# A fused attention and two MLPs in one kernel: the end of the attention, the first chunk of the first MLP, and the order inside an attention slot

## What is computed

```python
# q, k, v: (4, 8, 576, 64), s: (4, 8, 576)
scores = q @ k.T / sqrt(64)
cum    = cumsum(max(s, 0))
scores = where(causal, -1e9, scores + min(-(cum_i - cum_j), 0))
attn   = exp(scores - max) / (sum + 1e-9) @ v         # (4, 8, 576, 64)
x = attn as (2304, 512)
h = x @ w_in;  g = h - tanh(h);  x = g @ w_out         # w_in 512x2048, w_out 2048x512
h = x @ w2_in; solu = h * softmax(h)                   # w2_in 512x1024
out = layernorm(solu) * g_ln @ w2_out                  # w2_out 1024x512
```

## Time and profile before

| | us |
|---|---|
| median of 3 runs (lowest, highest) | 890.28 (888.71, 890.87) |
| the profiled execution | 890.16 |
| its span in the profile | 888.3 |
| PE busy | 851.2 (96%) |
| DVE busy | 445.8 (50%) |
| ACT busy | 381.2 (43%) |
| POOL busy | 104.1 (12%) |

### The profile page before, as it was taken

The page is one execution under the profiler, slowest core; times in us unless marked ns, Lnnn a source line. Parts: engine busy times, 40 slices in busy tenths (PEclk is TensorE's granted clock), DMA queues, the critical chain, the costliest instruction groups (busy, mean ns, idle before and its releaser), DMA issues.

```text
span 888.3 us, 14439 instructions
## 1 busy us (share of the span) xinstructions
PE 851.2 (96%) x4800; PEld 738.0 (83%) x4800; DVE 445.8 (50%) x1047; ACT 381.2 (43%) x856; POOL 104.1 (12%) x134
## 2 busy tenths in 40 slices
PE   4899999999979899999999999999999999999998
PEld 3788888888878678888888888899998888888886
DVE  4677877877743435222422322242565655544553
ACT  3777777777633334222322322232542433333332
POOL 2222222222100000000000000000003222112210
PEclk9899999999999999999999999999999999999999
DMA  6444444454303222000000000000210000000000
GB/s 153 120 123 122 121 128 128 118 141 112 117 31 95 71 95 95 1 1 1 0 0 0 0 0 0 0 0 1 60 36 0 25 24 24 12 24 24 24 24 35
DMA packets 77713, 46.28 MB, mean 52 GB/s; under 512 B 59824, under 2 KB 68144, under 8 KB 77680
## 3 DMA queue, kind: packets, MB, share of 16 engines
q1 hardware_dynamic: 77680, 45.86, 18.3%
HBM read 40.97 MB, written 4.87 MB: 52 GB/s over the span
## 4 chain that ended last, share of the span: by engine, by line
PE 78%; DVE 6%; DMA 4%; ACT 4%; issue 4%; SPq 1%; DVEq 0%; ACTq 0%
PE psum L1024 19%; PE psum L1011 19%; PE psum L1190 11%; PE psum L1218 11%; PE psum L1091 5%; PE psum L1051 4%; DMA stage<-in_moe_w_out 4%; PE psum L1119 4%; PE psum L1204 2%; PE psum L1055 1%; DVE probs L813 1%; ACT pT_hi L582 1%; DVE w1i L772 1%; DVE pT_lo L796 1%; ACT w1i L559 1%
## 5 line engine op out<-in xcount | busy, mean ns | idle before, releaser
L1011 PE MATMUL psum<-x_hi,w1i 128*128 128x464 f32 (+1 forms) x640 | 186.7, 373 | 4.8 <-DVE w1i L772 4.8
L1011 PEld LDWEIGHTS psum<-x_hi,w1i 128*128 128x128 f32 x640 | 120.8, 189 | 19.4 <-issue 3.5
L1011 PE MATMUL psum<-x_lo,w1i 128*128 128x464 f32 (+1 forms) x320 | 119.5, 373 | 0.0
L902 DVE TENSOR_TENSOR gate_lo<-gate,gate_hi 128x464 fp32r<-128x464 f32 (+1 forms) x80 | 51.1, 638 | 104.2 <-ACT gate_hi L667 103.4
L893 DVE TENSOR_TENSOR gate<-psum,gate 128x464 f32<-128x464 f32 (+1 forms) x80 | 51.0, 637 | 99.4 <-ACT gate L657 99.2
L667 ACT ACTIVATE gate_hi<-gate 128x464 fp32r<-128x464 f32 (+1 forms) x80 | 47.1, 588 | 113.0 <-PE psum L1024 102.3
L591 ACT ACTIVATE probs<-probs,neg_max 128x128 f32<-128x128 f32 (+2 forms) x144 | 83.8, 582 | 22.1 <-DVE neg_max L813 21.9
L1218 PE MATMUL psum<-w2o,lnT_hi 128*128 128x512 f32 x288 | 92.2, 401 | 0.5 <-DVE lnT_lo L971 0.5
L657 ACT ACTIVATE gate<-psum 128x464 f32<-128x464 f32 (+1 forms) x80 | 44.2, 553 | 109.4 <-PE psum L1011 107.3
L1024 PE MATMUL psum<-gate_hi,w1o_hi 128*128 128x464 f32 (+1 forms) x320 | 80.6, 373 | 8.1 <-DVE gate_lo L902 8.1
L582 ACT ACTIVATE pT_hi<-psum 128x512 fp32r<-128x512 f32 (+3 forms) x160 | 64.9, 438 | 42.9 <-PE psum L1119 42.9
(11 more groups left out here) (111 smaller groups left out, 1346.1 us busy)
## 6 DMA issues: line engine op xcount, KB each, us to landing
cum_bc<-cum_dram SPq DMA_DIRECT2D x16, 576.0 KB, 4.3
rden_T<-rden_dram SPq DMA_DIRECT2D x32, 144.0 KB, 2.9
out_x<-out_sb SPq DMA_DIRECT2D x18, 256.0 KB, 2.0
stage<-in_q SPq DMA_DIRECT2D x32, 128.0 KB, 2.3
stage<-in_k SPq DMA_DIRECT2D x32, 128.0 KB, 2.4
v_raw<-in_v SPq DMA_DIRECT2D x32, 128.0 KB, 3.6
stage<-in_moe_w_in SPq DMA_DIRECT2D x16, 256.0 KB, 2.7
stage<-in_moe_w_out SPq DMA_DIRECT2D x16, 256.0 KB, 3.0
```

Source lines behind the costliest of these rows:

```text
L902: dve.tensor_tensor(gate_lo[j % 2][:, 0:n], gate[j % 2][:, 0:n], gate_hi[j % 2][:, 0:n].bitcast(F32), ALU.subtract).then_inc(gate_lo_done, 1)
L1011: mm = pe.matmul(h_ps[j % 4][:, 0:wide(c)], wp[j][:, kt, :], xp[:, kt, 0:wide(c)], start=(n == 0), stop=(n == 3 * KT - 1))
```

## The change

The order and place of work change; what is computed does not.

- **Beginning.** k of pair 0 is issued from ACT's queue; SP issues s, q0, then cum's store, q1, the wait, cum_bc of pair 0, k1. DVE clears only the parts of `stage` ahead of the cumulative sums, the rest behind them. PE waits for four increments of dve_const. In slot -1 the three parts of q and k turn in three banks.
- **Slot order.** PE: `score(2)` ahead of `turn_rden`, `turn_qk(0)`. ACT: `exp(1, 0)`, `exp(1, 1)` ahead of `rden_rows_copy`, `qk_copy(0)`. DVE: `qk_rest(0)` behind `bias(0, 2)`, `bias(1, 2)`; `bias(None, FULL)` ahead of `qk_rest(2)`.
- **X_CUT** from 256 to 128.
- **Chunk 0.** `AHEAD = 4`. x of chunk 0 is split in halves at the ends of slots 14 and 15 (`first_x`); the four w_in tiles inside slot 16 (`first_w1i`); up(0, 0..3) inside and behind slot 16 (`first_up`). PE then runs down(j-4), up(j). step(0, 0) does not wait for the last x_mult. Steps 0 to 3 split two w_out tiles each, later ones tile j+4, and w_in tile j+3 behind gate_hi and gate_lo. The two halves of `stage` have a semaphore each; SP reloads each half by itself.
- Memory is laid out anew: `probs`, `qkT_hi`, `qkT_lo` and `cum_bc` come first, and the gates and the first w_out tiles lie on them.

```diff
-        AHEAD = 3
+        AHEAD = 4
-        HALF, X_CUT = S // 2, 2 * P
+        HALF, X_CUT = S // 2, P
+        def w1o_at(j):
+            return range(2 * j, 2 * j + 2) if j < AHEAD else range(j + AHEAD, min(j + AHEAD + 1, FT))
+        def qk_bank(sl, n):
+            return bank((5, 4, 3)[n]) if sl.fixed and sl.s < 0 else qk_ps
...
 # SP
-            for n in range(2):
-                load_qk(n, n)
+            load_tokens(sp, q_raw[0], q_pairs, 0, qk_in[0], diagonal=True)
             sp.wait_ge(cum_step, 3)
             sp.dma_start(cum_dram, cum8).then_inc(cum_out, 16)
+            load_tokens(sp, q_raw[1], q_pairs, 1, qk_in[1], diagonal=True)
             sp.wait_ge(cum_out, 16)
...
+                if sl.fixed and sl.s == -1:
+                    load_tokens(sp, k_raw[1], k_pairs, 1, qk_in[1])
                 if sl.fixed and sl.s == PAIRS - 1:
                     sp.wait_ge(turned_qk, 3 * PAIRS)
-                    for j in range(4):
-                        load_w1(j)
+                    for j in range(2):
+                        load_w1i(j)
...                                       # rden_T of this slot
+                if sl.fixed and sl.s == PAIRS - 1:
+                    for j in range(2, 4):
+                        load_w1i(j)
+                    for j in range(4):
+                        load_w1o(j)
...
             for j in range(4, FT):
+                sp.wait_ge(w1i_lo_done, j - 3)
+                load_w1i(j)
                 sp.wait_ge(w1o_lo_done, j - 3)
-                load_w1(j)
+                load_w1o(j)
...
 # ACT (DVE in the same places, with the lo parts)
+            load_tokens(act, k_raw[0], k_pairs, 0, qk_in[0])
+            def first_x(sl):
+                if sl.fixed and sl.s in (PAIRS - 2, PAIRS - 1):
+                    act.wait_ge(x_done, HALVES)
+                    split_x(0, (0, 1) if sl.s == PAIRS - 2 else (2, 3))
...
-            act.wait_ge(attended, 2 * PAIRS)
-            act.wait_ge(x_done, PAIRS)
+            act.wait_ge(turned_p, UNITS * PAIRS)
+            act.wait_ge(v_split, 2 * PAIRS)
             for j in range(FT):
+                if j == 1:
+                    act.wait_ge(x_done, PAIRS)
                 step(0, j)
...
 # DVE, end of a slot
                 p_lo("B2")
+                bias(None, FULL)
                 qk_rest(2)
-                bias(None, FULL)
+                first_w1i(sl, 3)
                 p_lo("B3")
-                ahead(sl)
+                first_x(sl)
+                if sl.fixed and sl.s == LAST:
+                    step(0, 0)
+                    x_mult()
...
 # PE
-            pe.wait_ge(dve_const, 2)
+            pe.wait_ge(dve_const, 4)
...
+                if weights:
+                    for j in range(AHEAD, FT):
+                        down(c, j - AHEAD, weights)
+                        up(c, j, weights)
+                    for j in range(FT - AHEAD, FT):
+                        down(c, j, weights)
...
                 turn_p("A2")
+                score(2)
                 turn_rden()
                 turn_qk(0)
-                score(2)
...
                 turn_qk(1)
+                if sl.fixed and sl.s == PAIRS:
+                    first_up(0)
...
                 attend(-1, 0, 1)
+                if sl.fixed and sl.s == PAIRS:
+                    first_up(1)
                 turn_p("B3")
                 attend(-1, 0, 2, 3, 4)
                 if sl.fixed and sl.s == PAIRS:
-                    pe.wait_ge(biased, TILES * PAIRS)
-                    up(0, 0, True)
+                    first_up(2)
             attention(pe, slot)
-            for j in range(1, AHEAD):
-                up(0, j, True)
+            first_up(3)
```

More of the change, by code:

```diff
@@ L165, in build_transformer @@
             gate_lo = [sb(f"gate_lo{n}", [P, CH], F32R) for n in range(2)]
+            w1o = sb("w1o", [P, FT, 2, DM], F32R)
+            w1o_hi, w1o_lo = ([w1o[:, j, part, :] for j in range(FT)] for part in range(2))
             sb("pad1", [P, pad])
@@ L191, in build_transformer @@
             w2o = sb("w2o", [P, FT2, 2, DM], F32R)
[L192 removed]
+            w2o_hi, w2o_lo = ([w2o[:, (f - AHEAD) % FT2, part, :] for f in range(FT2)] for part in range(2))
             y_hi = [sb(f"y_hi{n}", [P, KT, P], F32R) for n in range(2)]
@@ L225, in build_transformer @@
         stage_in = [sem(f"stage_in{n}") for n in range(4)]
+        w1o_in = [sem(f"w1o_in{n}") for n in range(4)]
         g_in = sem("g_in")
@@ new lines, in w2o_lo_part, with step @@
+            def w2o_lo_part(n):
+                for f in (2 * n, 2 * n + 1):
+                    dve.wait_ge(w2o_hi_done, f + 1)
+                    dve.scalar_tensor_tensor(out=w2o_lo[f][:, :], in0=stage[n][:, (f % 2) * DM:(f % 2 + 1) * DM],
+                                             scalar=g_col[:, f:f + 1], in1=w2o_hi[f][:, :].bitcast(F32),
+                                             op0=ALU.mult, op1=ALU.subtract).then_inc(w2o_lo_done, 1)
+            def step(c, j):
+                u = FT * c + j
+                dve.wait_ge(tanh_done, u + 1)
+                n = wide(c)
+                dve.tensor_tensor(gate[j % 2][:, 0:n], h_ps[j % 4][:, 0:n], gate[j % 2][:, 0:n],
+                                  ALU.subtract).then_inc(gate_done, 1)
+                if isinstance(c, int) and c == 0:
+                    for m in w1o_at(j):
+                        w1o_lo_part(m)
+                if isinstance(c, int) and c == NCH - 1 and FT2 <= j < FT2 + KT:
+                    w2i_lo_part(j - FT2)
+                if isinstance(c, int) and c == NCH - 1 and j >= FT2 + KT:
+                    w2o_lo_part(j - FT2 - KT)
+                dve.wait_ge(gate_hi_done, u + 1)
+                dve.tensor_tensor(gate_lo[j % 2][:, 0:n], gate[j % 2][:, 0:n], gate_hi[j % 2][:, 0:n].bitcast(F32),
+                                  ALU.subtract).then_inc(gate_lo_done, 1)
+                if isinstance(c, int) and c == 0 and 0 < j <= FT - AHEAD:
+                    w1i_lo_part(j + AHEAD - 1)
@@ L789, in slot, with first_x, first_w1i @@
+            def first_x(sl):
+                if sl.fixed and sl.s in (PAIRS - 2, PAIRS - 1):
+                    split_x(0, (0, 1) if sl.s == PAIRS - 2 else (2, 3))
+            def first_w1i(sl, j):
+                if sl.fixed and sl.s == PAIRS:
+                    w1i_lo_part(j)
             def slot(sl):
@@ L856, in slot @@
                 p_lo("A2")
-                qk_rest(0)
                 bias(0, 2)
                 bias(1, 2)
+                qk_rest(0)
+                first_w1i(sl, 0)
                 p_lo("A3")
-                x_mult()
+                if not (sl.fixed and sl.s == LAST):
+                    x_mult()
                 p_lo("T")
+                first_w1i(sl, 1)
                 qk_rest(1)
@@ L908, in copy_y @@
                     dve.tensor_copy(xT[:, m, tokens(c)], y_ps[m][:, 0:wide(c)]).then_inc(y_dve, 1)
-            for j in range(FT):
+            for j in range(1, FT):
                 step(0, j)
```

187 lines of the change are left out of this document (85 added, 102 removed).

## The result

| us | before | after |
|---|---|---|
| median (lowest, highest) | 889.77 (888.71, 890.87), 4 runs | 860.58 (860.31, 860.85), 4 runs |
| the profiled execution | 890.16 | 860.57 |
| its span | 888.3 | 858.7 |
| PE busy | 851.2 (96%) | 839.3 (98%) |

The ratio is 0.967, with a 95% interval of 0.966 to 0.969: 29.2 us less, where 22.6 were forecast. In what follows the spans of the two profiled executions are compared, 29.6 us apart.

What follows compares the result with a forecast made beforehand. PE, busy 96% of the span, was taken as the bound, with waits for gate_lo (8.1 us) and neg_max (7.1) to remove. 890.16 - 17.8 - 4.0 - 1.5 + 0.8 = 867.7 us; range 863.5 to 876.

Steps and rivals of the forecast that it cites:

- End of attention and chunk 0: Slot 16's start to chunk 1's first up: gaps, restart and half clock mostly go, gain 17.8 us, between 15.5 and 19.0.
- the tightest place: up(0, 4) in chunk 0, due at 24.0 with its tile ready at 23.8: 0.2 slack, 0.3 us taken.
- the residue of 1.2: Slot 16 and chunk 0: loss still left after the change, 0.9 us, taken as 1.2 with small latencies.
- Borders: Slot borders: PE's wait of about 0.3 us for neg_max of the tail tile goes, gain 4.0, ends 0 and 4.5.
- The other moves in the slot: Inside the slot: qk_lo(0) about 1.8 us later, rden_rows 1.3 later, both within slack; no gain or cost counted.
- X_CUT: Attends: key tile 1 saves 0.18 us, tile 0 costs 0.14; over 32 heads gain 1.5, ends 0 and 2.5.
- Beginning: Start through slot 0: PE starts about the same, slot 1 near 26.7 instead of 25.89; cost 0.8, ends -0.3 and 2.
- the swap's gain: Slot 0's end: the bias no longer waits behind qk_lo, saving 0.6 us against the new order's cost.
- the cost of the new order: Slot 0: turn_qk(1), at 18.43 before, waits for qk_lo(0) near 20.0 and pushes score(3); 1.4 us in the walk.
- The staging: Rival in chunk 0: SP's in-order queue keeps the 8.1 us of waits for gate_lo, 875.8 us; chance 11%.
- new wait: Rival in the slots: a stall at turn_qk(1) or T, 0.3 us a slot, eats the border gain, 871.7; 13%.
- The beginning did not stay longer at half clock: Rival: a thinner slot 0 moves the half clock past slot 1, +4 us, 871.7 us; chance 4%.

Runs made afterwards that it cites:

- the swap alone: The kernel before with one edit, DVE takes bias(None, FULL) ahead of qk_rest(2): 881.94 us, ratio 0.993.
- the two other traces with before's attention: The kernel before with w_out's parts side by side in memory, 888.73 us; the same with the gates also ahead of w1o, 888.04 us.
- the halves tied: The kernel after, but SP waits for both lo parts of a step before reloading either half of the staging tile: 860.39 us, ratio 0.969.
- the ups behind: The kernel after with up(0,0) to up(0,3) all behind the attention's last matmul, none inside slot 16: 862.24 us, ratio 0.971.
- the run of score(2) alone: The kernel before with score(2) ahead of turn_rden and turn_qk(0), ACT's and DVE's orders moved to match: 885.82 us, ratio 0.998.

## Why the prediction was right and wrong

- **End of attention and chunk 0: -17.8 forecast, -18.6 measured.** The account by waits held, though its parts were not run apart. Slot 16's start to chunk 1's first up is 92.1 (about 93 forecast), no wait for gate_lo or w_in is left, and up(0, 4), called the tightest place, starts at 250.59 with its tile ready near 250.0. Of the residue of 1.2, two waits are seen in slot 16: 0.48 for probs at its start and 0.18 for rden (0.5 and 0.6 forecast). The price of up(0, 4) and the small latencies did not come. One reading was off without harm: the earlier trace rows has ACT and DVE busy for 38% and 43% of chunk 0, not a third.
- **Borders: -4.0 forecast, -4.6 measured** over thirteen of the borders, 0.35 each. The mechanism, DVE's order of qk_lo and the tail's bias, is shown by the swap alone. The term was mis-sized because it was read from the idle column of PE. A matmul's shown end is modelled; the distance between starts is what counts, and it fell from 0.52 to 0.64 down to 0.21, by more than the 0.3 shown.
- **The other moves in the slot: nothing forecast, -4.6 measured.** This is the step that failed. The prediction asked of these moves only what they could harm ("rden_rows 1.3 later, used a slot after"), and never what stood where they were taken from. The waits of PE in 40 to 224 us held no more than 0.3 us for rden beside the earlier trace rows, so the place looked clean. In these thirteen slots the old order costs after 3.0 us, the new one gives before 4.5, and an early reciprocal alone gives before 3.9. After's 4.6 is thus about the order's 3.0 and the 1.65 that X_CUT by itself wins at the same place.
- The stall was in the profile, in the row beside. The waits of PE's weight loads (PEld) in slots 2 to 14 of before:

```profile
PEld psum L1051 <- DVE neg_max L813: 5.4, 20, 0.4
...
PEld psum L1144 <- issue: 2.6, 10, 0.6
PEld psum L1133 <- issue: 0.5, 3, 0.2
```

  L1144 is the turn of rden: ten times, once in each of slots 4 to 13, and "issue" because the profile finds no releaser for it. In after these three are gone. Together they are 8.5 us, near the 9.2 that borders and turn A2 gave; the matmul row showed 4.3. Not every wait in this list is a stall, though: two more rows of before, both "issue", have 8.0 us (mask, L1055) and 4.4 us (scores, L1051), and after has them unchanged. Only the comparison, or the releaser, tells which can be won. The Trainium skill (Perfetto Trace Analysis, "Identifying the Most-Contended Engine") says that matmul busy time is not a good measure of how close a kernel is to its limit, because pipelined instructions look smaller in the trace, and to go by the share of peak arithmetic and the busy share of the weight loads instead. This trace agrees: PE's matmuls were busy 97.6% of slots 2 to 14 (179.21 of 183.68), which leaves 4.5 us to win, the weight loads 86.3% (158.60), and the change won 9.9.
- **X_CUT: -1.5 forecast; -2.15 in thirteen slots by itself, -0.74 beside the other edits.** The size was near, the path was not: 1.65 of the 2.15 came from the stall of rden, and the attends, which were all that the forecast counted, give 1.0. The 0.11 that was taken for a 128-column matmul is not its columns' time: 64 columns take 0.11 too, as in slot 16 of after, where each matmul has a weight load of its own:

```profile
230.74 0.28 PE L1146 MATMUL psum<-pT_lo,v_hi 128*128 128x64 f32 x1
230.85 0.28 PE L1146 MATMUL psum<-pT_hi,v_lo 128*128 128x64 f32 x1
230.96 0.65 PE L1174 MATMUL psum<-ident,probs 128*128 128x128 f32 x4
```

  The weight loads between them start 0.11 apart too (230.71, 230.82), so a matmul this short costs its weight load. The Trainium skill (TensorE: Matmul & The Clock Gate, "LDWEIGHTS (loading the stationary operand)") gives columns / 1.2 ns for a load; for 128 columns that is an estimate of 107 ns, and this trace agrees. The formula that the prediction took from the same page of the Trainium skill ("Back-to-back issue gap") is for a matmul by itself, and the section says that it leaves the load out.
- **Beginning: +0.8 forecast, -0.17 measured** at the start of slot 2 in the two profiled executions, and the sign of that number is luck. The start at 7 us (7.44, for the clears) and the cost in slot 0 came as said: 13.46 against 12.25, slot 1 from 27.43 on, later than the 26.7 forecast. Slot 1 then took 12.62 against 14.33. But 14.33 is this one execution's: the two other traces with before's attention have 13.56 and 13.59 there and start slot 2 at 39.30 and 39.50, while after and the two kernels above that share its first slots (the halves tied, the ups behind) start it at 40.05, 39.80 and 39.97. By these the beginning costs 0.3 to 0.8, near the forecast. Of its two parts the swap's gain was priced at 0.6 and is at most 1.2 to 1.4, and the cost of the new order, 1.4 in the prediction's walk, is 1.6 to 1.8 by the run of score(2) alone; both readings carry a shift of the clock. A part of the difference inside slot 1 is the granted clock (same columns as the stretches above, 24 to 32 us, before and then after):

```profile
24.00:32.00 8.00, 6.11 (x36) 4.80 (x37) 4.43 (x18) 4.24 (x16) 2.19 (x4) 0.57 0.39 112
```

```profile
24.00:32.00 8.00, 6.31 (x42) 5.05 (x42) 5.23 (x21) 5.53 (x18) 1.32 (x2) 0.79 0.43 112
```

  A mean of 0.57 is 6.9 us at the half clock, 0.79 is 3.4. The column doesn't show all of it. The clock's records begin at 21.8 us in before and at 25.3 in after, what lies ahead of them is printed as 1.00, and there the lengths have to be read. The same matmuls at the end of slot 0, in before and then in after:

```profile
22.37 0.54 PE L1067 MATMUL psum<-qkT_hi 128*128 128x288 f32 x2
```

```profile
24.27 0.85 PE L1122 MATMUL psum<-qkT_hi 128*128 128x288 f32 x2
```

  So after ran at the half clock up to 25.3 and from 28.7 to 32.1, before up to 21.8 and from 25.2 to 32.0: 21.3 and 21.5 us from PE's first matmul on. After had as much of it, more in slot 0 and less in slot 1, so a part of slot 0's cost and of slot 1's gain is the same shift. What the order alone does to either slot was not parted from it.
- **The later chunks: no term, -0.73 measured.** The memory layout was left out of the sum. The runs show that it is the place of the gates and of w1o together; w1o's order alone does nothing.
- **The rivals.** The staging did not hold PE, with or without halves of their own. No new wait came in the slots; the slack at turn_qk(1) was enough. The beginning did not stay longer at half clock: 21.3 us against 21.5, over by 32.1 us in both.
- **The range** was too narrow downwards because every term's good end came from a wait that was seen; there was no room for a gain from a stall that the matmuls' waits hid.

## What to carry to other kernels

When operations change places in an engine's order, price the place they leave as well as the one they come to, from the distances between starts, not from the idle column: compare a stretch's length with the same work at its unstalled spacing, and read the weight loads' waits beside the matmuls'. An instruction that waits briefly for a neighbour engine in every turn of a loop is worth putting behind other ready work, even if the profile shows next to no wait for it. A buffer given back in two pieces gained nothing here, where one in-order queue reloads both. And before a difference at the beginning is put down to an edit, hold several traces of the same code side by side: slot 1 of before took 14.33, 13.56 and 13.59 in three of them.

## What was unexpected of the hardware

- A wait of PE cost more here than the time until its releaser was done: in before's slot 4 the turn of rden could have started at 70.66, the reciprocal was done at 70.92, and the turn started at 71.17; the instructions behind it started 0.22, 0.14 and 0.20 apart, and 0.11, 0.10 and 0.21 when rden was early. From 0.26 of waiting came 0.65 of delay.
- In this loop the same program's slots came out unequal in before (13.88 to 14.46), and equal to 0.06 once no such wait was left.
- At the beginning the clock column can't be trusted: before the first record of the clock (21.8 us in before, 25.3 in after) it prints 1.00, while the matmuls have the length of 1.2 GHz (four turns of 128 columns in 1.11 at 11.44, 0.45 later).
- The half clock of the beginning falls differently from trace to trace of the same code: with before's attention up to 21.8, 22.4 and 22.5 us, and then, from about the start of slot 1 on, for another 6.8, 3.4 and 3.4 us.
- Where the first MLP's tensors lie changes a matmul's spacing by 0.7 ns (81.01 against 80.75 us for 384). The cause is open.
